# One 128-partition DMA for q and k of a head, in an attention, routing and MLP kernel on one Trainium2 core

## The chip, the cores and the metric

The kernel runs on one core of one Trainium2 chip. The metric is the time of one execution on the device, in microseconds (us), as the median over runs. The engines are named as the profile names them: PE is TensorE's matmuls and PEld its weight loads, DVE is VectorE, ACT is ScalarE, POOL is GpSimd, SP is SyncE, which here issues DMAs only.

## What is computed

Windowed attention with a few sink keys, then a mixture of eight experts with top-1 routing, then a gated MLP, all in float32. Shapes: 4 batches, 8 heads, 768 positions, head width 64; 3072 tokens of width 512 behind it.

```
B, H, S, D = 4, 8, 768, 64          # n_sink 4, window 128
scores = q @ k^T / sqrt(D)          # kept where key < n_sink or 0 <= query - key < window
a = softmax(scores);  x = (a @ v) with the heads side by side      # 3072 x 512
e = argmax(x @ w_gate + modality_bias[modality_id])
x = gate(e) * (relu(x @ w1[e]) @ w2[e])                            # F = 1024
h = x @ w_in;  out = (h * sigmoid(1.702 h)) @ w_out                # 512 -> 2048 -> 512
```

## The kernel before

Each engine has its own program, written out by hand, and semaphores order them. The first stage, attention, takes batches in turn, in a batch the 8 heads, in a head 6 tiles of 128 queries: 192 steps. In a step TensorE makes the scores of a tile (L752 with k_hi, L753 with k_lo), VectorE adds the mask and finds the maximum (L1385), ScalarE takes exponentials (L1052), TensorE turns the probabilities (L764) and weighs the values (L789, L794), three and four steps later. Routing, the experts and the MLP follow from about 234 us on, bound by TensorE.

q and k come from DRAM already transposed, as `qkT[b, h]`, 64 rows (head width) of 2 x 768 numbers, q and k next to each other: 6144 contiguous bytes a row. They are wanted in both halves of the partitions, since a float32 product is made of rounded parts that stand above each other: partitions 0 to 63 and 64 to 127 of `qk_raw` get the same 64 rows. There are 4 slots of `qk_raw` (head modulo 4), each with its own semaphore `qk_loaded`.

GpSimd splits a head (`split_qk`: L577 to L587) into q_st, k_hi and k_lo; the first head is split by VectorE (`split_first`, L1251 to L1260) to start sooner. A split adds 3 to `qk_split`. The load of head h waits for the split of head h - 4, which had the same slot. TensorE waits for `qk_split` ahead of a head's first tile.

SyncE issues all loads of this stage from one queue. For each pair of heads that is done it stores x (`store_pair`, L399), loads vT three pairs ahead (L387), then v of the same pair of the next batch (`load_v`: one DMA of 128 partitions, L376, and four DMAs `v_sinks` of 4 partitions, L378), then q and k of two heads of the next batch, then one piece of w_in (`load_win`, L394).

GpSimd's program has the splits of all 31 heads first, and behind them the biases of the first three batches:

```
for h in range(1, B * H):
    split_qk(*divmod(h, SLOT))
...
pool.wait_ge(logits_added, B - 1)
pool.tensor_tensor(lg[:, 0:PRE, :], lg[:, 0:PRE, :], bias_of[:, 0:PRE, :], ALU.add).then_inc(pre_biased, 1)
```

VectorE takes part of the routing of these batches into the last batch's steps (`route_early(n)`, n from 0 to 47 for its tiles, so 33 lies in head 29 of 0 to 31):

```
if n == 33:
    dve.wait_ge(pre_biased, 1)
    dve.tensor_reduce(best[:, pre], lg[:, pre, :], AX.X, ALU.max).then_inc(best_found, 1)
```

TensorE begins with 28 matmuls of the identity (L844, `warm_up`), and has more of them in the first steps.

Of the kernel before, what the change touches and what calls it, by code (L numbers as in the profile page):

```python
# [40 lines left out]
def program(nc, qkT, vT, vP, modality, w_gate, bias, w1, w2, w_in, w_out, out, n_sink, window):  # L41
    B, H, D, _, S = qkT.shape
# [41 lines left out]
    SINK_ROWS = SINK_T * SINKS  # L84
    LOADS_V = 1 + SINK_T
    SLOT = 4
    LOADS_QK = 2
    LW, VW = 64, 80
    VEXT = D + 1 + E
    PRE = (B - 1) * QT  # L90
# [32 lines left out]
    with ExitStack() as ctx:  # L123
# [3 lines left out]
        def sem(name):  # L127
            return ctx.enter_context(nc.semaphore(name))
# [8 lines left out]
        def place(name, shape, dt=F32, at=None):  # L137

            at = top[0] if at is None else at
            at = -(-at // 8) * 8  # L140
            top[0] = at + int(np.prod(shape[1:]))
            assert top[0] <= arena_words, (name, top[0], arena_words)
            return nc.alloc_sbuf_tensor_at(name, shape, dt, offset=base + at * W4)
# [38 lines left out]
        qk_raw = place("qk_raw", [P, SLOT, 2, S], at=ZS)  # L182
# [97 lines left out]
        qk_loaded = [sem(f"qk_loaded{s}") for s in range(SLOT)]  # L280
# [85 lines left out]
        def _(sp):  # L366
            def load_qk(b, h):

                slot = h % SLOT
                for half in range(2):  # L370
                    sp.dma_start(qk_raw[half * D:half * D + D, slot], qkT[b, h]).then_inc(qk_loaded[slot], 16)

            def load_v(b, c):

# [27 lines left out]
            for c in range(PAIRS):  # L402
                sp.sem_inc(x_stored[c], DMA)
            load_qk(0, 0)
            load_qk(0, 1)
            load_vt(0)
            sp.wait_ge(cleared, 3)
            for half in range(2):
                sp.dma_start(wg_sb[half * D:(half + 1) * D, :, half * E:(half + 1) * E],
                             w_gate.rearrange("(c h d) e -> h d c e", h=2, d=D)[half]).then_inc(wg_loaded, 16)  # L410
            load_v(0, 0)
            load_qk(0, 2)
            load_qk(0, 3)
            load_vt(1)
# [99 lines left out]
        def _(pool):  # L514
# [50 lines left out]
            def split_qk(r, slot):  # L565

                g = r * SLOT + slot
                pool.wait_ge(qk_loaded[slot], r * (LOADS_QK * 16) + LOADS_QK * 16)
                if r:
# [650 lines left out]
        def _(dve):  # L1220
# [23 lines left out]
            def split_first():  # L1244

                dve.wait_ge(qk_loaded[0], LOADS_QK * 16)
                raw_q, raw_k = qk_raw[:, 0, 0, :], qk_raw[:, 0, 1, :]
# [461 lines left out]
```

## Time and profile before

| | |
|---|---|
| median of 3 runs | 1119.26 us (1118.54 to 1119.34) |
| profiled execution | 1117.76 us |
| its span, first to last instruction | 1115.8 us |
| TensorE's mean granted clock | 0.998 |
| PE busy | 1100.6 us (99%) |
| DVE, ACT, POOL busy | 424.8, 377.8, 326.1 us |
| DMA queue q1 (SyncE's) | 51584 packets, 72.56 MB |
| q/k loads | 64 issues of 384 KB, median 8.2 us to landing |

Busy time is a sum of instructions' spans; matmuls are pipelined, so a busy PE is not PE at its peak. A wait costs time only where the waiting engine is on the path that ends last. The DMA figures are means over 16 DMA engines.

### The profile page before, as it was taken

To read this page: it belongs to the slowest core of one execution; us is meant where nothing else is said; L and a number is where in the kernel's file an instruction comes from. 1 tells how busy PE (TensorE), PEld (TensorE's weight loads), DVE (VectorE), ACT (ScalarE), POOL (GpSimd) and SP (SyncE) were. 2 spreads that over 40 slices of the span, in tenths; PEclk is the share of its full clock that TensorE was granted. 3 is DMA by queue.
4 is the path that set the end of the run, shared out by engine and by line. 5 is a ranking of instruction groups with operands and counts; after the bars stand their busy time and mean duration, and the time that the engine had idled before them with its cause. 6 is when DMAs were issued, how large, how long until landed. Compare 5 with 4: busy or idle time off the path is not lost.

```text
span 1115.8 us, 18740 instructions
## 1 busy us (share of the span) xinstructions
PE 1100.6 (99%) x5952; PEld 942.0 (84%) x5953; DVE 424.8 (38%) x1089; ACT 377.8 (34%) x781; POOL 326.1 (29%) x441
## 2 busy tenths in 40 slices
PE   9999999999999999999999999999999999999998
PEld 9999999987888888888878888888888888888887
DVE  5566666685122233212264223223223222322222
ACT  3666666643222233222344222222222222222222
POOL 8888888645641212212121001001001001000100
PEclk9999999999999999999999999999999999999999
DMA  9999999237111133211142001001001000000101
GB/s 222 217 258 236 239 229 229 72 124 264 38 47 47 47 108 127 75 47 38 38 147 89 20 1 56 19 0 47 27 1 47 19 9 28 9 0 1 38 1 38
DMA packets 57392, 92.04 MB, mean 82 GB/s; under 512 B 7936, under 2 KB 32768, under 8 KB 57344
## 3 DMA queue, kind: packets, MB, share of 16 engines
q1 hardware_dynamic: 51584, 72.56, 24.3%
q0 software_dynamic: 5760, 18.89, 4.8%
q8 instruction: 24, 0.39, 0.2%
q14 instruction: 24, 0.20, 0.1%
HBM read 72.02 MB, written 19.41 MB: 82 GB/s over the span
## 4 chain that ended last, share of the span: by engine, by line
PE 91%; DVE 4%; ACT 2%; issue 2%; DMA 1%; ACTq 0%; DVEq 0%; POOL 0%; SPq 0%; POOLq 0%
PE psum L981 8%; PE psum L982 8%; PE psum L983 8%; PE psum L972 8%; PE psum L974 8%; PE psum L973 8%; PE psum L789 5%; PE psum L938 4%; PE psum L940 4%; PE psum L913 4%; PE psum L915 4%; PE psum L914 4%; PE psum L939 4%; PE psum L764 2%; PE psum L925 2%
## 5 line engine op out<-in xcount | busy, mean ns | idle before, releaser
L1643 DVE TENSOR_TENSOR g<-psum,g 128x512 f32<-128x512 f32 x96 | 66.3, 691 | 295.0 <-ACT g L1176 295.0
L1176 ACT ACTIVATE g<-psum 128x512 f32<-128x512 f32 x96 | 57.4, 598 | 307.5 <-PE psum L974 304.0
L972 PE MATMUL psum<-x2T,win_hi 128*128 (+1 forms) x384 | 149.6, 390 | 2.3 <-DVE g L1643 2.3
L981 PE MATMUL psum<-w_hi,gT_hi 128*128 128x512 f32 x384 | 151.3, 394 | 0.0
L983 PE MATMUL psum<-w_hi,gT_lo 128*128 128x512 f32 x384 | 149.6, 390 | 0.0
L982 PE MATMUL psum<-w_lo,gT_hi 128*128 128x512 f32 x384 | 149.6, 389 | 0.0
L974 PE MATMUL psum<-x2T,win_lo 128*128 (+1 forms) x384 | 149.5, 389 | 0.0
L973 PE MATMUL psum<-x2T,win_hi 128*128 (+1 forms) x384 | 149.4, 389 | 0.0
L721 POOL DMA_INDIRECT out<-o_out,out_rows x20 | 21.5, 1075 | 412.6 <-ACT o_out L1189 408.1
L789 PE MATMUL psum<-v_sb,pT 128*128 128x73 f32 x704 | 105.9, 269 | 2.4 <-DVE pT L1397 1.2
L1385 DVE CUSTOM_DVE_ANT_0 s_msk<-psum,mask_sb 128x260 f32<-128x260 f32 (+1 forms) x192 | 75.0, 403 | 70.6 <-PE psum L753 38.2
L789 PEld LDWEIGHTS psum<-v_sb,pT 128*128 128x128 f32 x704 | 93.4, 191 | 8.9 <-DVE pT L1397 7.6
L1052 ACT ACTIVATE probs<-s_msk,negmax 128x260 f32<-128x260 f32 (+1 forms) x192 | 93.5, 494 | 13.9 <-DVE negmax L1385 13.7
L1646 DVE TENSOR_TENSOR gT_lo<-g,gT_hi 128x512 fp32r<-128x512 f32 x96 | 66.5, 693 | 65.9 <-ACT gT_hi L1180 65.9
L972 PEld LDWEIGHTS psum<-x2T,win_hi 128*128 128x128 f32 x384 | 72.1, 188 | 17.6 <-issue 2.7
L913 PE MATMUL psum<-w_hi,xsT_hi 128*128 128x512 f32 x208 | 83.2, 400 | 2.2 <-DVE xsT_lo L1582 2.2
L1180 ACT CAST gT_hi<-g 128x512 fp32r<-128x512 f32 x96 | 59.6, 620 | 75.7 <-DVE g L1643 75.7
L983 PEld LDWEIGHTS psum<-w_hi,gT_lo 128*128 128x128 f32 x384 | 72.1, 188 | 15.2
L974 PEld LDWEIGHTS psum<-x2T,win_lo 128*128 128x128 f32 x384 | 72.1, 188 | 14.9
L973 PEld LDWEIGHTS psum<-x2T,win_hi 128*128 128x128 f32 x384 | 72.1, 188 | 14.9
L982 PEld LDWEIGHTS psum<-w_lo,gT_hi 128*128 128x128 f32 x384 | 72.2, 188 | 14.4
L981 PEld LDWEIGHTS psum<-w_hi,gT_hi 128*128 128x128 f32 x384 | 72.1, 188 | 14.4
(229 smaller groups left out, 1988.5 us busy)
## 6 DMA issues: line engine op xcount, KB each, us to landing
qk_raw<-qkT SPq DMA_DIRECT2D x64, 384.0 KB, 8.2
stage<-w SPq DMA_DIRECT2D x12, 1024.0 KB, 6.8
x<-y_rows SPq DMA_DIRECT2D x24, 256.5 KB, 2.7
vT_sb<-vT SPq DMA_DIRECT2D x16, 384.0 KB, 9.4
v_sb<-vP SPq DMA_DIRECT2D x16, 384.0 KB
x_rows<-x_sb SPq DMA_DIRECT2D x16, 384.0 KB, 5.7
win_raw<-w_in SPq DMA_DIRECT2D x16, 256.0 KB, 10.3
stage<-w_out SPq DMA_DIRECT2D x4, 1024.0 KB, 6.6
```

The costliest lines, as they stand in the source:

```text
L789: mm = pe.matmul(o, pT[:, n % 2, k * P:(k + 1) * P], v_sb[:, c, kb, half * VEXT:(half + 1) * VEXT], start=(i == 0 and k == 0), stop=(k == ...
L913: pe.matmul(psum[:, HB[hf], :], xsT_hi[:, c, :], hi, start=(c == 0), stop=False)
L972: pe.matmul(bank, wh, hi, start=(c == 0), stop=False)
L973: pe.matmul(bank, wh, lo, start=False, stop=False)
L974: mm = pe.matmul(bank, win_lo[:, c, f * P:(f + 1) * P], hi, start=False, stop=(c == CH - 1))
L981: pe.matmul(psum[:, OB[t], :], gh, hi, start=(f == 0), stop=False)
L982: pe.matmul(psum[:, OB[t], :], gh, lo, start=False, stop=False)
L983: return pe.matmul(psum[:, OB[t], :], gT_lo[:, f % 4, t * P:(t + 1) * P], hi, start=False, stop=(f == F2C - 1))
L1052: act.activation(probs[:, n % RING, 0:width[i]], s_msk[:, n % RING, 0:width[i]], ACT.Exp, bias=negmax[:, n % 8:n % 8 + 1], scale=-1.0).the ...
L1385: dve.tensor_tensor_reduce(s_msk[:, n % RING, 0:width[i]], psum[:, S_ps[n % 3], 0:width[i]], mask_sb[:, min(i, MASKS - 1), 0:width[i]], -S ...
L1643: dve.tensor_tensor(g32[:, f % 2, :], psum[:, FB[f % 2], :], g32[:, f % 2, :], ALU.mult)\
L1646: dve.tensor_tensor(gT_lo[:, f % 4, :], g32[:, f % 2, :], gT_hi[:, f % 4, :].bitcast(F32), ALU.subtract).then_inc(gT_split, 1)
```

## The change

Instead of two DMAs of 64 partitions for a head there is one of 128, whose source names the 64 rows twice by an outer step of 0. The semaphore count of a loaded head goes from 32 to 16 with it.

```
-    LOADS_QK = 2
+    LOADS_QK = 1
...
             def load_qk(b, h):
 
                 slot = h % SLOT
-                for half in range(2):
-                    sp.dma_start(qk_raw[half * D:half * D + D, slot], qkT[b, h]).then_inc(qk_loaded[slot], 16)
+                both = qkT[b, h].rearrange("(o d) w s -> o d (w s)", o=1).broadcast_to([2, D, 2 * S])
+                sp.dma_start(qk_raw[:, slot].rearrange("p w s -> p (w s)"), both).then_inc(qk_loaded[slot], 16)
```

Only SyncE's list of instructions differs. At the head of its program, shapes are those of the destination (partitions first); the source of the new DMA is 2 (step 0) x 64 x 1536, that of the old one 64 x 1536:

```order
-L371 DMA qk_raw<-qkT 64x1536 x4
+L371 DMA qk_raw<-qkT 128x1x1536 x2
 L387 DMA vT_sb<-vT 128x768
 L409 DMA wg_sb<-w_gate 64x4x8 x2
 L376 DMA v_sb<-vP 128x6x128
 L378 DMA v_sinks<-vP 4x128 x4
-L371 DMA qk_raw<-qkT 64x1536 x4
+L371 DMA qk_raw<-qkT 128x1x1536 x2
```

Every pair of q/k issues has become one in its place, 64 in all before and 32 now; nothing else has moved on any queue.

## Rows read from the trace of the kernel before

**Rows 1.** The page: busy time, and DMA in 40 slices of the span.

```profile
PE 1100.6 (99%) x5952; PEld 942.0 (84%) x5953; DVE 424.8 (38%) x1089; ACT 377.8 (34%) x781; POOL 326.1 (29%) x441
...
DMA  9999999237111133211142001001001000000101
GB/s 222 217 258 236 239 229 229 72 124 264 38 47 47 47 108 127 75 47 38 38 147 89 20 1 56 19 0 47 27 1 47 19 9 28 9 0 1 38 1 38
```

**Rows 2.** Waits, 0 to 220 us: total, times, longest.

```profile
POOL q_st L577 <- DMA qk_raw<-qkT: 13.7, 9, 2.8
...
PEld psum L789 <- DVE pT L1397: 6.5, 24, 0.8
...
DVE q_st L1251 <- DMA qk_raw<-qkT: 3.0, 1, 3.0
```

**Rows 3.** Instructions that read q_st: ns min/median/max, first and last start.

```profile
L752 PE MATMUL psum<-k_hi,q_st x192: 305/367/508, 10.7 to 229.3; 128*128 128x260 f32 x160, 128*128 128x128 f32 x32
```

**Rows 4.** The DMA view, 0 to 220 us: packets, issues.

```profile
DMA packets 37278, 47.47 MB, mean 216 GB/s; under 512 B 6016, under 2 KB 29312, under 8 KB 37248
...
qk_raw<-qkT SPq DMA_DIRECT2D x64, 384.0 KB, 8.2
vT_sb<-vT SPq DMA_DIRECT2D x16, 384.0 KB, 9.4
v_sb<-vP SPq DMA_DIRECT2D x16, 384.0 KB
x_rows<-x_sb SPq DMA_DIRECT2D x14, 384.0 KB, 7.2
win_raw<-w_in SPq DMA_DIRECT2D x14, 256.0 KB, 10.4
v_sinks<-vP SPq DMA_DIRECT2D x64, 2.0 KB
wg_sb<-w_gate SPq DMA_DIRECT2D x2, 8.0 KB, 7.2
mod_i<-modality SPq DMA_DIRECT2D x1, 24.0 KB, 5.0
bias_sb<-bias SPq DMA_DIRECT2D x1, 8.0 KB, 3.6
```

**Rows 5.** The DMA view, 235 to 270 us, 40 slices (expert weights).

```profile
GB/s 0 0 0 13 292 172 9 26 129 407 412 396 398 398 232 0 159 141 0 73 187 400 403 384 407 400 407 309 26 0 0 0 75 267 307 412 386 377 389 403
```

**Rows 6.** Windows at the start: busy time of each engine, PEclk, DMA share, GB/s.

```profile
2.00:3.00 1.00, 1.00 (x6) 1.00 (x6) 1.00 (x1) 0.54 (x2) 0.71 (x3) 1.00 0.70 178
4.00:7.00 3.00, 3.00 (x16) 3.00 (x15) 0.13 (x3) 0.00 (x0) 2.08 (x8) 1.00 1.02 225
7.00:10.00 3.00, 3.00 (x28) 3.00 (x27) 2.84 (x5) 0.00 (x0) 2.81 (x10) 1.00 0.98 220
10.00:13.00 3.00, 3.00 (x29) 3.00 (x28) 2.69 (x13) 0.15 (x1) 2.77 (x8) 1.00 1.21 290
```

**Rows 7.** Timeline of TensorE at the start (start, duration).

```profile
1.80 9.12 PE L844 MATMUL psum<-ident 128*128 128x128 f32 x56 [1.80 <-POOL ident L526]
```

**Rows 8.** Timeline of GpSimd: its last split, and the biases behind it.

```profile
202.51 0.82 POOL L577 CAST q_st<-qk_raw 128x768 fp32r<-128x768 f32 x1 [0.37 <-issue]
...
208.00 0.23 POOL L586 TENSOR_TENSOR k_lo<-qk_raw,k_hi 128x24 fp32r<-128x24 f32 x1
...
211.06 0.49 POOL L606 TENSOR_TENSOR lg<-lg,bias_of 128x144 f32<-128x144 f32 x1
```

**Rows 9.** Timeline of VectorE: the reduction at step 33 of the last batch.

```profile
214.06 0.30 DVE L1358 TENSOR_REDUCE best<-lg 128x18 f32<-128x144 f32 x1
```

**Rows 10.** Windows behind attention, columns as in rows 6.

```profile
244.00:246.00 2.00, 2.00 (x20) 2.00 (x20) 1.77 (x7) 0.19 (x1) 0.00 (x0) 1.00 1.05 406
247.00:249.00 2.00, 2.00 (x12) 2.00 (x11) 2.00 (x3) 1.28 (x2) 1.23 (x1) 0.50 0.41 151
```

**Rows 11.** Timeline of TensorE, 241 to 246 us.

```profile
243.02 2.82 PE L879 MATMUL psum<-tile_tok,oh_slot 128*128 128x32 f32 x24 [1.07 <-DVE tile_tok L1487]
```

## The prediction

> **What bounds the kernel now.** I read the page first. TensorE is busy for 1100.6 us, 99% of the span, and its clock is full [rows 1, 6]. So a change to loads can lose time without limit, but win only what TensorE spends waiting. The slices show one stage that differs: in the first seven (0 to 195 us, attention) the 16 DMA engines are 0.9 busy and move 217 to 258 GB/s [rows 1].
>
> Then the waits of that stage. GpSimd waits 13.7 us in nine pieces for q and k, VectorE once, 3.0 us, for the first head; of TensorE's own waits the longest in total is 6.5 us, on the moved probabilities, and no row of that view has it wait for q or k [rows 2]. So today q and k arrive in time. The first score matmul starts at 10.7 us and the last of 192 at 229.3 [rows 3]: 218.6 / 191 = 1.145 us a step, 6.87 us a head. GpSimd's split of a head takes 202.51 to 208.23, 5.7 us [rows 8].
>
> **What the change does to the loads.** A head brings 2 x 384 KB = 786,432 bytes (exactly 2 x 64 rows x 6144) in either form; HBM is read twice for both. What differs is how the bytes are dealt to the DMA engines. The new source is a loop of 2 (step 0) over 64 rows over 1536 elements; its destination counts 128 partitions. The two halves can be cut apart; any finer cut would have to run through the loop of 2.
>
> What does the trace say about dealing? Count the packets under 512 bytes in 0 to 220 us: 6016 [rows 4]. Data account for 3072 (modality, 128 x 24 of 8 bytes), 512 (w_gate, 2 x 64 x 4) and 128 (bias): 3712. The other 2304 are completion writes. The 128 DMAs besides v_sinks, at 16 each, make 2048, which leaves 256 for the 64 v_sinks DMAs: 4 each, and those are the DMAs with 4 rows. A DMA is dealt along its outermost count, one completion per engine used: 64 or 128 rows go to 16 engines, 4 rows to 4. By that, a source with 2 outermost goes to 2 engines, each with 64 packets of 6144 bytes = 393,216 bytes. No row has a DMA whose two sides count differently, so this step is inference; I hold it at about 9 in 10.
>
> The Trainium skill ("DMA: Bandwidth & Descriptors", the section on the semaphore increment of 16) states it outright: the number of engines is the largest up to 16 that divides the slowest count of both sides; its rules for kernel authors warn of just this form, a leading zero-stride broadcast. By that rule the load has 2 engines. The trace's four completions per four-row DMA agree with it.
>
> **The price of a load.** One engine's best rate: streams to all 128 partitions reach 412 GB/s in a slice of 35/40 us [rows 5], 412 / 16 = 25.75 GB/s an engine. At that, 393,216 bytes take 15.27 us, against 6.87 us in which a head is consumed. Four slots cover latency, not a rate that is 2.2 times too low. Today's half loads are slower: in 4 to 7 us nearly nothing but q and k moves, at 225 GB/s [rows 6], 14.1 an engine; but there 16 engines write into one half, here each half has one. I take 25.75, and keep 14.1 (28.0 us a load) as the far bound. 32 x 15.27 = 488.6 us.
>
> **What else is in the two engines.** I assume that one queue is served in order. Ahead of the last q/k load SyncE issues 16 v_sb, 15 vT, 12 x_rows (384 KB each) and 11 win_raw (256 KB). v_sb and x_rows go in pieces of 512 bytes: 28 x 393,216 = 11.01 MB, priced at 290 GB/s from the stretch 10 to 13 us with v in it [rows 6], 38.0 us. vT and win_raw, 8.78 MB, at the 406 of the weight loads [rows 10], 21.6 us. v_sinks puts 32 KB on each of four engines, 1.8 us at 18.1 GB/s. Sum 61.4; all at 412 GB/s it would be 48. No gap is added: the load of head h waits for the split of head h-4, 5.7 us after a landing, while three more loads (46 us) are in flight; the wait of SyncE for finished heads ahead of each x_rows store concerns heads six or more back. Of 64 issues 32 fall away on SyncE; that gains nothing, as the DMA engines are late, not SyncE.
>
> First packets move at about 2.1 us (the stretch from 2 to 3 us is 0.70 busy; estimated) [rows 6]. The last q/k load lands at 2.1 + 488.6 + 61.4 + 1 (its completion, estimated) = **553 us**; today the last split starts at 202.5.
>
> **What is late next.** Not simply the last head. GpSimd splits all heads and only then makes the biases of batches 0 to 2; VectorE waits for that (pre_biased) at step 33 of the last batch, which is head 29, not 31. So VectorE, and TensorE with it, stands there until head 31 has landed, been split, and the biases are done: 202.51 to 211.55, 9.04 us [rows 8]. In the trace VectorE comes to that point at 214.06 [rows 9], 2.5 us after GpSimd; this cover goes. Behind it lie 14 steps, two heads, and routing, all unchanged. VectorE's row moves from 214.06 to 553.1 + 9.1 = 562.2: a shift of 348.1 us.
>
> **Clock.** At the start 16 ident matmuls begin in the 3 us up to 7 and 28 in the next 3 [rows 6], and at 247 to 249 us the granted clock is 0.50 (1.2 GHz) with 6 matmuls a us, some us after an idle stretch of 1.07 us [rows 10, 11]. With 10 us idle per head TensorE will fall to that level in attention. During the loads that is hidden: even doubled, a head is 13.7 us against 17.2. Only the restart at step 33 shows it: today's first 5.4 us at half pace lose 2.7; I take 3, between 0 and 16 (14 steps doubled).
>
> **Sum.** The profiled execution took 1117.8 us (span 1115.8 and 2 around it), 1.5 below the median of 1119.3, well inside the 0.2% (2.2 us) that a measurement here can tell. 1117.8 + 348.1 + 3 = **1469 us**. Everything behind attention costs what it costs now.
>
> **Rivals.**
> - *Sixteen engines after all* (the pattern is flattened to 128 rows on its way). The load becomes a whole-width stream: 786,432 bytes at 406 GB/s [rows 10], 1.9 us. For it: the destination has 128 rows, and v_sb with 128 has 16 completions. The 13.7 us of GpSimd and the 3.0 of VectorE vanish. Neither is on the path: TensorE is never released by them [rows 2], and at the start TensorE's own warm-up matmuls fill the time up to the first score matmul: they run from 1.80 to 10.92, that one starts at 10.7 [rows 3, 7]. Time 1118, no change. It decides once the load is dealt to six engines or more: 393,216 x 2 / 6 at 25.75 GB/s is 5.1 us, plus 1.9 of other traffic, about the 6.87 of a head. The Trainium skill ("SBUF — State Buffer", on the DMA port swizzle) says that 64 partitions reach half the ports, so whole-width loads go faster; the rows agree, 225 [rows 6] against 406 [rows 10]. By that alone the change would relieve DMA, and it would still end at 1118.
> - *Two engines, and slow ones.* If an engine keeps the 14.1 GB/s of the half loads, a load takes 28.0 us and 32 take 896: 1469 + 407 = 1876. Against it: one writer per half.
> - *Hidden by the prefetch.* Excluded by the rate above: the queue has no slack over 200 us to lend.
> - *The clock does not return by itself* after step 33: 1469 + 13 = 1482, inside the range.
>
> **How the numbers follow.** Two engines at the full rate 0.83; two slow engines 0.05; sixteen engines 0.10, of which 0.02 faster by over 0.2% (a start brought forward); others, such as four or eight engines, 0.02. The predicted time is the first. Its own range: 48 for other traffic gives 1456, and an engine that is 5% faster when 14 others are idle takes another 24, to 1432; the lower slices of the same streams, 384 to 386 GB/s [rows 5], give 24.1 an engine and 33 more, and the clock up to 13, to 1515. 1430 to 1520 holds that, some 8 in 10 of all. Faster 0.02, same 0.08, slower 0.90.
>
> **What would show it.** Right: the DMA share in attention falls to about 2/16 = 0.12 plus little, some 50 GB/s of q and k; packets keep their count of 6144-byte pieces while completion writes fall by 64 x 16 - 32 x 2 = 960 (fewer packets under 512 bytes); a q/k load lands 45 to 65 us after issue; GpSimd waits about 11 us per head; the first score matmul moves from 10.7 to about 22 (head 0 lands at about 18, not at 7); the step rate becomes 17 us a head; VectorE's `best` row is at about 560, held by GpSimd; the rest of the span is as long as it was after 214. Wrong: a DMA share near 0.9 or bursts of 400 GB/s with landings of 2 to 4 us (sixteen engines), or a load every 28 us (the far bound). The prediction falls most easily at its inference from four-row DMAs to a looped source.

## The result, and the profile after

The changed kernel takes 1485.4 us (median of 5 runs, 1484.28 to 1489.99), the kernel before 1118.9 in the same set: ratio 1.3282, interval 1.3266 to 1.3298. The profiled execution took 1489.99 us, with a span of 1488.2. Where runs of one kernel lie more than 1.5% above its fastest, they are named apart below and comparisons go by the others.

The page of the changed kernel: busy time, 40 slices of now 37 us, the count of packets, and the chain by engine; behind it the count of packets on the page of the kernel before.

```profile
PE 1196.0 (80%) x5952; PEld 1029.8 (69%) x5953; DVE 424.9 (29%) x1089; ACT 377.8 (25%) x781; POOL 324.0 (22%) x441
...
PEclk7666666666666665999999999999999999999999
DMA  1122222222222222441114211410100001000000
GB/s 65 70 74 84 78 84 84 89 78 84 88 87 95 80 84 67 152 146 48 42 42 155 71 42 35 163 29 1 42 14 35 21 0 49 7 28 0 29 1 29
DMA packets 56432, 92.03 MB, mean 62 GB/s; under 512 B 6976, under 2 KB 31808, under 8 KB 56384
...
PE 61%; SPq 19%; DMA 11%; issue 4%; POOL 2%; DVE 2%; ACT 0%; ACTq 0%; POOLq 0%; DVEq 0%
```

```profile
DMA packets 57392, 92.04 MB, mean 82 GB/s; under 512 B 7936, under 2 KB 32768, under 8 KB 57344
```

Set against [rows 1]: the slices of attention have grown from 7 to 16, their DMA share has fallen from 0.9 to 0.2 and their rate from 217 to 258 down to some 84 GB/s. That is not less work but fewer engines at it: the bytes are the same. TensorE's clock row, full everywhere before, stands at 0.6 to 0.7 in the same slices. DVE, ACT and POOL are busy for as long as before. On the page of before the count under 512 bytes is 7936; here it is 6976, 960 fewer. Those are the completion writes that are gone: 64 loads x 16 before, 32 x 2 now.

Windows of the changed kernel (busy time by engine, PEclk, DMA share, GB/s):

```profile
3.00:10.00 7.00, 6.67 (x52) 6.48 (x51) 1.13 (x5) 0.00 (x0) 4.43 (x22) 1.00 0.12 47
...
50.00:55.00 5.00, 2.57 (x20) 2.29 (x19) 1.87 (x10) 1.47 (x4) 1.67 (x3) 1.00 0.13 53
...
100.00:200.00 100.00, 55.13 (x325) 51.89 (x323) 25.91 (x123) 25.99 (x75) 31.59 (x35) 0.67 0.25 82
...
411.50:421.50 10.00, 2.42 (x10) 2.12 (x10) 1.44 (x7) 1.27 (x4) 5.52 (x6) 0.64 0.13 53
...
579.00:591.00 12.00, 10.50 (x47) 10.20 (x48) 5.95 (x31) 3.77 (x12) 5.79 (x18) 0.50 0.00 0
591.00:597.00 6.00, 5.68 (x45) 5.37 (x44) 4.93 (x23) 3.96 (x13) 1.94 (x4) 0.93 0.41 112
```

Where q and k alone move, or nearly (3 to 10, 50 to 55, 411.5 to 421.5 us), the share is 0.12 and 0.13, that is 2 of 16 engines, at 47 to 53 GB/s; [rows 6] had 1.02 and 225. The last two rows are for the clock, below.

Waits of the changed kernel, 0 to 600 us (total, times, longest):

```profile
POOL q_st L577 <- DMA qk_raw<-qkT: 363.8, 29, 26.3
...
PE psum L809 <- issue: 146.3, 14, 11.5
...
PE psum L752 <- POOL k_lo L586: 81.7, 14, 7.1
...
DVE best L1358 <- POOL lg L606: 27.3, 1, 27.3
POOL q_st L577 <- PE psum L753: 27.2, 2, 13.6
...
DVE q_st L1251 <- DMA qk_raw<-qkT: 15.5, 1, 15.5
```

GpSimd's 13.7 us in nine waits [rows 2] have become 363.8 in 29, 12.5 each, and TensorE, which never waited for q or k, now does, through GpSimd. Rows from the view of q_st and from the timelines of GpSimd and VectorE give the end of the stage:

```profile
L752 PE MATMUL psum<-k_hi,q_st x192: 305/473/840, 22.9 to 597.6; 128*128 128x260 f32 x160, 128*128 128x128 f32 x32
...
535.43 0.82 POOL L577 CAST q_st<-qk_raw 128x768 fp32r<-128x768 f32 x1 [10.62 <-DMA qk_raw<-qkT]
...
570.77 0.82 POOL L577 CAST q_st<-qk_raw 128x768 fp32r<-128x768 f32 x1 [10.01 <-DMA qk_raw<-qkT]
...
579.28 0.48 POOL L606 TENSOR_TENSOR lg<-lg,bias_of 128x144 f32<-128x144 f32 x1
...
579.80 0.30 DVE L1358 TENSOR_REDUCE best<-lg 128x18 f32<-128x144 f32 x1 [27.34 <-POOL lg L606]
```

The score matmuls run from 22.9 to 597.6 instead of 10.7 to 229.3 [rows 3]. Two heads are 570.77 - 535.43 = 35.3 us apart. The last split starts at 570.77 (202.51 before, [rows 8]), the reduction `best` at 579.80 (214.06, [rows 9]), now held for 27.34 us by GpSimd's biases. From there to the end of the span it is 1488.2 - 579.8 = 908.4 us, before 1115.8 - 214.1 = 901.7. So of the 372.4 us between the two spans 365.7 are in front of this one row and 6.7 behind it.

### The profile page after: what moved, and what is told of

It is laid out like the page before. It is cut to its first block, busy times and chain, and to the rows that moved or that the text cites. A ratio compares the mean times of both kernels' runs of the same rounds, so it can differ in the third digit from the quotient of the medians.

```text
span 1488.2 us, 18708 instructions
## 1 busy us (share of the span) xinstructions
PE 1196.0 (80%) x5952; PEld 1029.8 (69%) x5953; DVE 424.9 (29%) x1089; ACT 377.8 (25%) x781; POOL 324.0 (22%) x441
## 2 busy tenths in 40 slices
DMA packets 56432, 92.03 MB, mean 62 GB/s; under 512 B 6976, under 2 KB 31808, under 8 KB 56384
## 4 chain that ended last, share of the span: by engine, by line
PE 61%; SPq 19%; DMA 11%; issue 4%; POOL 2%; DVE 2%; ACT 0%; ACTq 0%; POOLq 0%; DVEq 0%
DMA qk_raw<-qkT 10%; PE psum L981 6%; PE psum L983 6%; PE psum L982 6%; PE psum L972 6%; PE psum L973 6%; PE psum L974 6%; SPq L387 5%; SPq L394 4%; SPq L376 4%; PE psum L913 3%; PE psum L914 3%; PE psum L915 3%; PE psum L938 3%; PE psum L940 3%
## 5 line engine op out<-in xcount | busy, mean ns | idle before, releaser
L752 PE MATMUL psum<-k_hi,q_st 128*128 128x260 f32 (+1 forms) x192 | 89.9, 468 | 113.0 <-POOL k_lo L586 81.7
L809 PE MATMUL psum<-wg_sb,vT_sb 128*128 128x64 f32 x192 | 46.1, 413 | 155.5 <-issue 146.3
L809 PEld LDWEIGHTS psum<-wg_sb,vT_sb 128*128 128x128 f32 x192 | 44.1, 329 | 159.5 <-issue 150.1
L1077 ACT COPY pT<-psum 128x256 f32<-128x256 f32 (+1 forms) x160 | 56.0, 350 | 362.9 <-PE psum L764 360.9
L789 PE MATMUL psum<-v_sb,pT 128*128 128x73 f32 x704 | 131.2, 317 | 11.1 <-issue 8.9
L789 PEld LDWEIGHTS psum<-v_sb,pT 128*128 128x128 f32 x704 | 124.0, 246 | 15.4 <-issue 9.3
L752 PEld LDWEIGHTS psum<-k_hi,q_st 128*128 128x128 f32 x192 | 47.9, 250 | 118.6 <-POOL k_lo L586 83.8
L577 POOL CAST q_st<-qk_raw 128x768 fp32r<-128x768 f32 x31 | 25.5, 822 | 391.0 <-DMA qk_raw<-qkT 363.8
L764 PE MATMUL psum<-ident,probs 128*128 128x128 f32 x352 | 87.3, 329 | 0.1
## 6 DMA issues: line engine op xcount, KB each, us to landing
vT_sb<-vT SPq DMA_DIRECT2D x16, 384.0 KB, 21.3
```

What stands on the lines that cost most here:

```text
L752: pe.matmul(s, q, k_hi[:, slot, at:at + width[i]], start=True, stop=False)
L764: mm = pe.transpose(bank[:, k * P:(k + 1) * P], probs[:, n % RING, k * SEG:k * SEG + P], ident[:])
L789: mm = pe.matmul(o, pT[:, n % 2, k * P:(k + 1) * P], v_sb[:, c, kb, half * VEXT:(half + 1) * VEXT], start=(i == 0 and k == 0), stop=(k == ...
L809: pe.matmul(psum[:, VW_ps, t * LW:(t + 1) * LW], vT_sb[:, g % 2, t * P:(t + 1) * P], wg_sb[:, c, :], start=True, stop=True)
```

## The experiments

Ten kernels ran. Each is the changed kernel but for the lines shown, unless said otherwise; the lines of run 6 are set against the kernel before. Medians of the kernel before beside them were 1118.4 to 1118.9.

**1. The loop of 2 behind the rows.**

```
-both = qkT[b, h].rearrange("(o d) w s -> o d (w s)", o=1).broadcast_to([2, D, 2 * S])
+both = qkT[b, h].rearrange("d (o w) s -> d o (w s)", o=1).broadcast_to([D, 2, 2 * S])
```

> The loop of 2 (step 0) goes behind the rows: the source is 64 rows x 2 copies x 1536, so that a row lands in two neighbouring partitions instead of in the two halves (q and k stand in other partitions, the output is not the reference's). Bytes, packets, broadcast, number of issues and semaphore count are those of the change. Theory A (the number of engines follows the outermost count of both sides): 16 engines, attention bound by TensorE again, 1116 to 1120 us, DMA waits of GpSimd under 14 us, first head in by 5 us. Rival B (reading a row twice in one DMA, or one large DMA per head, is what is slow): 1450 to 1490 us, as the changed kernel.

1117.6 us, ratio 0.9992 (0.9982 to 1.0001): all of the loss is gone. Its rows, the window of the start and the DMA issues:

```profile
3.00:10.00 7.00, 7.00 (x56) 7.00 (x56) 4.43 (x11) 0.00 (x0) 5.41 (x23) 1.00 1.01 336
...
qk_raw<-qkT SPq DMA_DIRECT2D x32, 768.0 KB, 6.2
```

Share 1.01 and 336 GB/s where the change had 0.12 and 47, with the same bytes, the same broadcast and the same 32 issues. There is also a landing time again (6.2 us), where the page of the changed kernel has none for q and k. Packets under 512 bytes are 7425 on its page: 449 more than the 6976 of the changed kernel, where 32 loads with 16 completions instead of 2 make 448. Rival B is out.

**2 and 3. Four and eight outermost.** n is 4 or 8:

```
+rows = qkT[b, h, 0:2 * D // n]
+both = rows.rearrange("(o d) w s -> o d (w s)", o=1).broadcast_to([n, 2 * D // n, 2 * S])
```

> The source is 4 copies (step 0) of the first 32 rows, so the data of rows 32 to 63 are left out (the output is not the reference's); bytes and packets per load stay. Theory A: 4 engines, 32 packets of 236 ns each, 7.6 us a load and 1.9 us of other traffic, 9.5 to 9.8 us a head. Last q/k load at about 310 to 318 us, VectorE's row best at 319 to 327, time 1225 to 1240 us. DMA share in attention about 0.3. Rival B (broadcast or size of the DMA): 1450 to 1490 us.

> The source is 8 copies (step 0) of the first 16 rows, the other rows are left out (the output is not the reference's). Theory A: 8 engines, 16 packets each, 3.8 us a load and 1.9 us of other traffic, 5.7 us against 6.87 in which a head is consumed: just enough, 1118 to 1126 us. Rival B: 1450 to 1490 us. A rival C, in which loss is proportional to the load's duration without a threshold: 2 engines lose 366 us at 15.3 us a load, so 3.8 us would lose 91, 1210 us.

Four: 1265.8 us (three runs, 1265.4 to 1274.0), and 1285.8 in a fourth, which is the profiled one. Eight: 1172.7 and 1185.8 us (the second is profiled), and two longer runs of 1202.3 and 1206.9. In the order of theory A, and its sizes wrong both times. Count of packets, window of the start, two windows with q and k alone and last split of each, four first:

```profile
DMA packets 56497, 92.04 MB, mean 72 GB/s; under 512 B 7041, under 2 KB 31873, under 8 KB 56449
...
3.00:10.00 7.00, 7.00 (x50) 7.00 (x49) 1.13 (x5) 0.00 (x0) 4.43 (x22) 1.00 0.50 101
...
66.00:71.00 5.00, 3.19 (x26) 2.87 (x24) 2.46 (x12) 2.58 (x8) 0.00 (x0) 1.00 0.26 69
75.00:80.00 5.00, 4.84 (x24) 4.87 (x25) 0.44 (x2) 1.27 (x4) 4.84 (x6) 0.50 0.25 103
...
368.35 0.82 POOL L578 CAST q_st<-qk_raw 128x768 fp32r<-128x768 f32 x1 [3.98 <-DMA qk_raw<-qkT]
```

```profile
DMA packets 56624, 92.04 MB, mean 78 GB/s; under 512 B 7168, under 2 KB 32000, under 8 KB 56576
...
3.00:10.00 7.00, 6.73 (x53) 6.54 (x51) 1.13 (x5) 0.00 (x0) 4.46 (x22) 1.00 0.89 148
...
12.00:17.00 5.00, 1.51 (x7) 1.51 (x8) 4.00 (x16) 0.27 (x1) 0.00 (x0) 0.81 0.48 108
...
79.00:83.00 4.00, 4.00 (x21) 4.00 (x21) 1.06 (x4) 0.79 (x3) 1.63 (x2) 0.50 0.52 123
...
269.99 0.82 POOL L578 CAST q_st<-qk_raw 128x768 fp32r<-128x768 f32 x1
```

The counts give the number of engines: the 7936 of before less its 1024 completions of q and k, and 32 loads with 4 or 8 completions on top, make 7040 and 7168 (7041 and 7168 on the pages).

The windows of the start hold other loads too (shares of 0.50 and 0.89, where 4 and 8 engines of 16 are 0.25 and 0.50), so no rate of an engine comes out of them. With q and k alone, at shares of 0.25 to 0.26 and 0.48 to 0.52, four engines move 69 or 103 GB/s, 17 or 26 an engine, depending on the stretch, and eight 108 to 123, 13.5 to 15.4 an engine. A head takes (368.35 - 25.02) / 30 = 11.4 us with four and (269.99 - 19.08) / 30 = 8.4 with eight (25.02 and 19.08 are the first splits by GpSimd in their timelines), where 9.5 and 5.7 were expected; the 11.4 is from the longest of its four runs, and by the spans the others would have some 0.7 less (an estimate). Eight engines at 25.75 would have been enough. At 108 to 123 GB/s a load takes 7.3 to 6.4 us, and with 1.9 of other traffic that is 9.2 to 8.3, above 6.87 and of the size of the 8.4 measured. What slows them is asked in runs 6, 7 and 8.

Rival C is out by run 1: at 336 GB/s a load there takes 2.3 us, for which it would lose some 55 us (366 x 2.3 / 15.3), and run 1 loses none.

**4. q and k twice in DRAM.**

```
+"qkT": np.ascontiguousarray(np.stack([np.stack([q.transpose(0, 1, 3, 2), k.transpose(0, 1, 3, 2)], axis=3)] * 2, axis=2)),
...
+both = qkT[b, h].rearrange("o d w s -> (o d) (w s)")
```

> q and k stand twice in DRAM, so one DMA of 128 distinct rows loads a head, with the layout and all results of the kernel. Theory A: 16 engines over both halves, first head in by 5 us, loads of 2 to 4 us when alone, waits of GpSimd for q and k under 5 us; but TensorE was not released by them before, and its warm-up fills the start, so 1116 to 1119 us, not told apart from before. A rival, that the half loads cost attention time through the DMA queue (v, vT or x late): 1105 to 1114 us.

1118.6 us, ratio 0.9997 (0.9987 to 1.0007). One DMA of 128 rows costs nothing and brings nothing. Start and DMA issues:

```profile
3.00:10.00 7.00, 7.00 (x50) 7.00 (x50) 4.44 (x11) 0.00 (x0) 5.40 (x22) 1.00 0.96 330
...
qk_raw<-qkT SPq DMA_DIRECT2D x32, 768.0 KB, 5.9
```

The q/k waits of GpSimd on DMA are no longer among the waits, the slices of attention reach 398 GB/s, and the time stays.

**5. Routing moved ahead of the last two splits.**

```
-for h in range(1, B * H):
+for h in range(1, B * H - 2):
     split_qk(*divmod(h, SLOT))
 (the block from the biases to tiles_seen)
+for h in range(B * H - 2, B * H):
+    split_qk(*divmod(h, SLOT))
```

> The changed kernel, with GpSimd's block of biases and early routing moved ahead of the splits of heads 30 and 31 (all results kept). Theory A (two engines pace attention, and VectorE's wait for the biases adds the 14 steps behind step 33 to the last landing): the last split stays at about 571 us, VectorE's best row comes about 30 us earlier with no long wait, the last score matmul falls from 597.6 to 583 or 585, time 1470 to 1473 us. Rival D (the end of attention is set by something else after the last landing): 1483 to 1487 us.

1478.5 us: 6.9 less than 1485.4, half of what was expected, but beyond the spread (1477.2 to 1479.4 against 1484.3 to 1490.0). Score matmuls, last split and two windows:

```profile
L755 PE MATMUL psum<-k_hi,q_st x192: 305/474/840, 23.1 to 589.2; 128*128 128x260 f32 x160, 128*128 128x128 f32 x32
...
571.20 0.82 POOL L577 CAST q_st<-qk_raw 128x768 fp32r<-128x768 f32 x1 [4.94 <-DMA qk_raw<-qkT]
...
571.00:577.00 6.00, 3.29 (x16) 3.32 (x17) 0.00 (x0) 1.27 (x4) 5.54 (x6) 0.50 0.20 68
577.00:583.00 6.00, 6.00 (x33) 5.79 (x33) 2.23 (x11) 0.95 (x4) 0.00 (x0) 0.60 0.00 0
583.00:589.00 6.00, 5.56 (x48) 5.21 (x47) 5.25 (x26) 4.13 (x13) 2.35 (x5) 1.00 0.41 112
```

The last split starts where it did (571.20 against 570.77), `best` now runs at 552.3, and the last score matmul comes 8.4 us earlier. So the wait for the biases was on the path. The rows put the other half of the gain on the clock of the head that remains: PEclk is 0.50 and 0.60 up to 583, and from the end of its split to its last score matmul it takes 589.2 - 576.9 = 12.3 us, where a head before took 6.87.

**6. Two engines, both in one half.**

```
+rows = qkT[b, h, 0:D // 2].rearrange("(o d) w s -> o d (w s)", o=1).broadcast_to([2, D // 2, 2 * S])
+for half in range(2):
+    sp.dma_start(qk_raw[half * D:half * D + D, slot].rearrange("p w s -> p (w s)"), rows).then_inc(qk_loaded[slot], 16)
```

(with LOADS_QK = 2)

> Two DMAs per head, one for each partition half, each with 2 copies (step 0) of the first 32 rows (rows 32 to 63 are left out, the output is not the reference's). By theory A each runs on 2 engines, 64 packets an engine and head, as in the changed kernel; but now both engines write into the same half at a time, 32 partitions apart. If an engine's pace depends on what other engines write to the same half (theory P, also read into the 8-engine run, whose packets took longer), packets take 400 to 470 ns, a load 26 to 30 us, time 1750 to 1950 us. If not (theory Q: 236 ns a packet whoever else writes), 1470 to 1500 us.

1495.4 us (two runs), 10 above the changed kernel: as theory Q by its time, but not by its first window. Windows of this kernel, then of the changed one:

```profile
3.00:10.00 7.00, 7.00 (x47) 7.00 (x47) 1.13 (x5) 0.00 (x0) 4.46 (x22) 1.00 0.12 32
10.00:20.00 10.00, 0.76 (x7) 0.56 (x6) 0.00 (x0) 0.00 (x0) 0.00 (x0) 0.69 0.14 47
```

```profile
10.00:20.00 10.00, 0.00 (x0) 0.00 (x0) 0.32 (x1) 0.00 (x0) 0.00 (x0) 0.75 0.24 85
```

At the start both engines are equally busy (share 0.12) but move 32 GB/s instead of 47, 16 an engine; then 47. The first head is in at 23.9 us instead of 19.7, later loads keep pace with the changed kernel's. Perhaps two engines that begin in step on partitions 32 apart hinder each other until they are out of step; that is a guess from the windows, and no run tests it.

**7 and 8. What slows eight engines.**

```
+both = qkT[b, :, 0:16].rearrange("h d w s -> h d (w s)")          # 8 x 16 rows, all different
```

```
+rows = qkT[b, h, 0:8]                                             # 16 x the same 8 rows
+both = rows.rearrange("(o d) w s -> o d (w s)", o=1).broadcast_to([16, 8, 2 * S])
```

> As the run with 8 copies of 16 rows, but each of the 8 parts of the load is 16 rows of another head (step of a head, not 0), so that no row is read twice in a load (most rows of q and k are left out, the output is not the reference's). Destination, engines, packets and bytes are those of the 8-copy run. Theory R (several engines reading the same rows at once is what made its packets slow): packets back at 236 ns, 5.7 us a load with the other traffic, attention bound by TensorE, 1118 to 1126 us, last score matmul at about 230 us. Theory W (it is the writing side: which partitions the 8 engines fill at one time): as the 8-copy run, 1170 to 1207 us, last score matmul at about 290 to 300 us.

> The source is 16 copies (step 0) of the first 8 rows (the other rows are left out, the output is not the reference's): 16 engines that write as in the run with doubled q and k, but all read the same 8 rows. Theory R: packets slower than 234 ns, loads of 6 us or more, waits of GpSimd for q and k, 1125 to 1250 us. Theory W: as the run with q and k doubled in DRAM, 1116 to 1120 us.

Eight with different rows: 1173.7 us (two runs, 1169.0 and 1178.5), score matmuls to 280.6. Sixteen with the same rows: 1118.7 us, ratio 1.0001. Windows of the start, and with q and k alone, in this order:

```profile
3.00:10.00 7.00, 7.00 (x45) 7.00 (x45) 1.13 (x5) 0.00 (x0) 4.42 (x22) 1.00 0.89 159
...
11.00:16.00 5.00, 0.78 (x3) 0.79 (x4) 3.70 (x14) 0.00 (x0) 0.00 (x0) 0.83 0.50 120
```

```profile
3.00:10.00 7.00, 7.00 (x49) 7.00 (x49) 4.18 (x11) 0.00 (x0) 5.48 (x21) 1.00 0.99 245
...
21.00:23.00 2.00, 1.45 (x13) 1.21 (x12) 1.11 (x5) 1.26 (x4) 2.00 (x3) 1.00 1.03 227
```

Eight engines stay slow without any row read twice (120 against 108 to 123 GB/s with q and k alone, and a time as in the shorter runs of run 3), so the reading of the same rows is not their main trouble. But sixteen engines on the same eight rows move 245 GB/s in the window of the start where sixteen on different rows moved 330: that costs something too, as theory R said, but the attention stage does not feel it, and the time is theory W's. For the eight engines theory R is out as the main cause; that the writing side slows them (theory W) is what is left of the two, and no run shows it by itself.

**9 and 10. A shorter warm-up.** WARM_UP = 4 instead of 7, in the kernel of run 4 and in the kernel before.

> The kernel with q and k doubled in DRAM and 4 instead of 7 rounds of warm-up matmuls. If the start is held by the warm-up there (first head in by 5 us, split by 9), the first score matmul starts 1 to 1.5 us earlier, 1117 to 1118 us; if TensorE's clock comes up later for want of the three rounds, 1118 to 1121 us.

> The kernel before with 4 instead of 7 rounds of warm-up, the control of the run above: head 0 is split at 10.5 us, so the start stays at 10.5 to 10.7 us, 1118 to 1120 us, with an idle gap of some 4 us ahead of the first score matmul, which may cost clock.

With q and k doubled: 1117.05 us, ratio 0.9982 (0.9974 to 0.9991), first score matmul at 9.0 us. In the kernel before: 1120.2, ratio 1.0010 (1.0002 to 1.0019). Its windows:

```profile
7.00:10.00 3.00, 0.86 (x8) 0.67 (x6) 2.83 (x5) 0.00 (x0) 2.81 (x10) 0.99 0.98 209
10.00:13.00 3.00, 2.47 (x11) 2.48 (x12) 2.52 (x12) 0.14 (x1) 2.77 (x8) 0.50 1.18 297
```

There TensorE is idle for 2.67 us ahead of the first score matmul, the granted clock then stands at 0.50, and `best` comes at 216.9 instead of 214.1. The whole load is worth 0.2% only together with a warm-up that ends when it lands; that kernel has the lowest median here.

## Why the prediction was right, step by step

- **TensorE bound, q and k in time, nothing to win.** Run 4 shows it: loads of full width, no change.
- **Two engines.** Shown by share 0.12 to 0.13, 960 fewer completion writes, and run 1, which changes nothing but the order of the source's loops. The inference from DMAs of four rows held. By the rule of the Trainium skill ("DMA: Bandwidth & Descriptors", the section on the semaphore increment of 16) an outermost 64 and 128 give 16 engines, and 2 and 128 give 2. The completions counted agree for 2 (the change), 4, 8 and 16 (runs 2, 3 and 1).
- **15.27 us a load and 1.92 of company, 17.2 us.** Measured (570.77 - 19.7) / 31 = 17.8 (19.7: VectorE starts on head 0). This 3% is the largest miss, 18 us by the end: the last split starts at 570.8, not 553. In the windows with q and k alone, 47 to 53 GB/s are 23.5 to 26.5 an engine, around the 25.75 taken; in the middle of the stage it is 52 to 53, 14.8 to 15.1 us a load. So the load was sized well, and the short term is the other traffic: some 2.7 to 2.9 us a head instead of 1.92. It falls on every second head: from 412 us on the splits are by turns 15.7 to 16.9 and 19.3 to 19.7 us apart. No run tries its parts one by one.
- **No gap.** That held, and its reason did not: three more loads were to be in flight, and a load was to land 45 to 65 us after its issue. SyncE, held up by its own issues, gives out a pair of heads at about the time at which the pair ahead has landed:

```profile
499.46 2.46 SPq L371 DMA_DIRECT2D qk_raw<-qkT  x2
...
535.48 2.26 SPq L371 DMA_DIRECT2D qk_raw<-qkT  x2
```

  Head 29 is split at 535.43; heads 30 and 31, issued at 535.48, are split at 555.08 and 570.77, so they land at most 20 and 36 us behind that. As far as the shares tell, the engines do not run dry by it: of the stretches of 1 us from 5 to 569 us none has a DMA share under 0.09 and nine are under 0.12 (a share does not say which engines are busy). GpSimd waited twice, 27.2 us in all, for a slot that TensorE had not freed; these two splits come 19.3 us behind the one ahead, as their neighbours of the same turn do.
- **First score matmul at 22.** It came at 22.9.
- **GpSimd's biases hold step 33.** 9.04 us were expected from the last split to the biases' end and to `best`; measured 579.80 - 570.77 = 9.03. Run 5 shows that the wait cost time.
- **Clock.** 3 us taken, 6.7 measured behind `best`. The windows show 0.50 for 12 us from 579 on, up to 591, where the start [rows 6] had suggested 5.4 us at half pace. That half pace was read from the count of matmuls alone; PEclk in the same rows reads 1.00. The term was under-sized, and it also made run 5's expectation of the gain too large. That all of the 6.7 is clock is not shown.
- **Sum.** 348.1 + 3 predicted, 365.7 + 6.7 measured: 1469 against 1490 for the profiled execution and 1485 for the median.
- **Rivals.** Slow engines at 14.1 GB/s did not come: one writer per half kept 23.5 to 26.5. But their idea, that an engine's pace depends on the others, came back with eight engines (13.5 to 15.4 GB/s each), and so the point that I gave for the change to cost nothing, "six engines or more", fell: eight cost 54 us in the shortest run and 88 in the longest.

## What to carry to other kernels

Look at the outermost count of both sides of a DMA, and, in a stretch where nothing else moves, at whether the DMA share is a round fraction of 16: a broadcast put in front of the rows made one tidy DMA out of two and took 14 of 16 engines away. Merging two issues wins nothing where the engines were in time; if it is wanted, keep the rows outermost or let DRAM hold the second copy. When a stage becomes late, look for what its engines have queued behind the late work: here biases of other batches, one line behind the last split, held the last two heads.

## What was not expected of the hardware

- SyncE's issues grow long. Those of q and k took 0.5 to 2.2 us before, and the longest of the stage, one of v_sinks, 4.2; now many issues last 11 to 14 us, and the chain gives SyncE 19%. Two rows of its timeline:

```profile
466.32 12.19 SPq L394 DMA_DIRECT2D win_raw<-w_in  x1
...
482.15 13.60 SPq L376 DMA_DIRECT2D v_sb<-vP  x1
```

  In the chain it looks like the cause, but with 16 engines per load (run 1) the same list of issues has its longest q/k issue at 3.6 us, and in the changed kernel the DMA share never falls by much under that of two busy engines (above). So the long issues go with the busy engines; what holds an issue is not shown. vT then comes late (21.3 us from issue to landing, 9.4 before [rows 4]), and TensorE waits 146 us in all at L809, which by the program waits for vT; the view names no releaser there.
- The rate is not in proportion to the number of engines. With q and k alone 2 engines moved 47 to 53 GB/s, 4 moved 69 to 103, 8 moved 108 to 123 (120 on different rows); 16 moved 330 to 336 in the window of the start. Two engines in one half moved 32 in that window, in two halves 47.
- From 555 to 579 us TensorE was busy for 1.9 us. It then ran 12 us at the granted clock of 0.50, the 1.2 GHz level, busy for 10.5 of them, before the clock rose to 0.93 in the window from 591 on.
